# A tile of the fullest expert between the dense stage and the routed one, experts in another order, and another engine waiting for the last stores

## The chip, the cores and the metric

The kernel runs on 1 core of one Trainium2 chip. Its metric is device time in microseconds (us) of one execution. Engines are called PE or TensorE (matmuls), VectorE or DVE, ScalarE or ACT, GpSimd or POOL, and SyncE or SP (which here issues DMAs only).

## The reference

Linear attention without a softmax (4 batches, 8 heads, 576 rows, 64 columns) gives x of 2304 rows by 512. A dense mixture of 4 experts follows, then a routed one of 8 experts with one expert a row:

```python
    for e in range(E):                       # dense: E = 4, F = 1024
        h = np.maximum(x @ w1[e], 0.0)
        out += p[:, e:e + 1] * (h @ w2[e])
...
    logits = xn @ en.T / tau                 # routed: E = 8, F = 1024
    expert_idx = np.argmax(logits, axis=1)
...
    for e in range(E):
        mask = expert_idx == e
        h = np.maximum(x[mask] @ w1[e], 0.0)
        out[mask] = gate_w[mask, None] * (h @ w2[e])
```

By this formula on its inputs (seed 0) the 8 experts get 120, 639, 189, 727, 149, 36, 293 and 151 rows; of the first 1536 rows the fourth expert gets 484.

## The kernel before, in words

Every product keeps nearly full precision by splitting both sides into a high part (fp32r) and the remainder: high times high, high times low and low times high, three matmuls (`three`, L1285).

**Dense stage.** 48 steps (`STEPS`): 3 thirds of 768 rows by 16 units (4 experts by 4 quarters of F). A step's `up` has seven products (a Strassen-like scheme, combined on VectorE in `combine`), then `down` makes six tiles of 128 rows, which VectorE adds to the accumulator `acc` (`add`, L976). GpSimd makes the low parts of the weights. Meanwhile the routed weights are split "ahead" (steps in `AHEAD_AT`) and stored as `parts` in HBM: for each expert eight pieces of 1 MB, four of w1 and four of w2 (`PIECE`, `PCS`).

**Routing.** The 18 tiles of rows are routed in 7 blocks (`BLOCKS`); 4 blocks of 3 tiles inside the dense steps (`ROUTE_AT`), and 3 blocks of 2 in the tail, while the last third's down products run in the order `TAIL`. For a tile: PE transposes it (`flip`, L1367), ScalarE takes the squares (`route`) and copies the transposed rows to `xt`, PE makes logits (`logits`, L1382, one tile at a time; or, inside the steps, `logits_by_tile` and `logits_by_token`, L1392 and L1403, three tiles together), GpSimd the norms (`norms`), VectorE the one-hot (`choose`, L1033), ScalarE the exponentials, PE the rank of each row within its expert (`ranks`, L1414 to L1418), VectorE each row's place (`place`), and GpSimd scatters the rows with an indirect DMA (`scatter`, L551) into `rows` in HBM, a region for each expert.

**Tables.** When all 18 tiles are ranked, VectorE works out tables from the counts (L1112 to L1152): which row each tile begins at (`tab_r`, L1133, first `tab_ready`), which place (expert in use) it belongs to (`tab_o`, L1141, second), the expert of each place and the tiles through each place (third). SP loads two numbers (L410) and issues the rows of tiles 0 and 1 (L413). PE runs small matmuls on the identity in between (`WARM`, L1517, L1520, L1524).

**Routed stage.** A loop over pairs of tiles, as many as the tables say (rounded up to a pair). For a tile PE transposes the rows (`flip_rows`, L1465), multiplies by w1 (`routed_up`, 24 matmuls), transposes the hidden rows (`flip_hidden`, L1499) and multiplies by w2 (`routed_down`, 24). ScalarE and VectorE split what is transposed (`rx`, `rt_parts`, L825, L835, L1158, L1170), VectorE multiplies by the gate (`results`), and GpSimd stores with an indirect DMA (`store`, L615) and fetches the rows of a later tile (`load_rows`, L601). SP loads the weights into two slots, the place's w1 when the last up product of the place two before it is done, and its w2 after its last down product (`load_matrix`, L400). At the end GpSimd waits for the stores:

```python
            for s in range(2):
                pool.wait_ge(stored[s], 16 * ((tiles + 1) // 2))
```

Every engine ends with a closing DRAIN and a barrier, which the profile puts at line 198.

## Time and profile before

| | us |
|---|---|
| median of 3 runs | 1143.15 |
| lowest, highest | 1142.08, 1145.65 |
| profiled execution, its own time | 1145.34 |
| its span, first to last instruction | 1143.8 |
| PE busy | 1119.3 (98%) |
| DVE, POOL, ACT busy | 728.7, 655.3, 456.9 |
| HBM read, written | 170.99 MB, 79.98 MB |

Times in the rows count from the start of the span. "L1112" is line 1112 of the kernel. An idle time in brackets stands with what ended it. Starts of merged rows are those of the first instruction, and matmul ends are modelled, so neighbouring matmuls overlap.

### The profile page before, as it was taken

To read this page: it belongs to the slowest core of one execution; us is meant where nothing else is said; L and a number is where in the kernel's file an instruction comes from. 1 tells how busy PE (TensorE), PEld (TensorE's weight loads), DVE (VectorE), ACT (ScalarE), POOL (GpSimd) and SP (SyncE) were. 2 spreads that over 40 slices of the span, in tenths; PEclk is the share of its full clock that TensorE was granted. 3 is DMA by queue.
4 is the path that set the end of the run, shared out by engine and by line. 5 is a ranking of instruction groups with operands and counts; after the bars stand their busy time and mean duration, and the time that the engine had idled before them with its cause. 6 is when DMAs were issued, how large, how long until landed. Compare 5 with 4: busy or idle time off the path is not lost.

```text
span 1143.8 us, 18712 instructions
## 1 busy us (share of the span) xinstructions
PE 1119.3 (98%) x6210; PEld 985.1 (86%) x6211; DVE 728.7 (64%) x1160; ACT 456.9 (40%) x812; POOL 655.3 (57%) x609
## 2 busy tenths in 40 slices
PE   8999999999999999999999999999989999999996
PEld 8888899998899888999898888999887888888885
DVE  4867888888866788888866788888662222222221
ACT  4783444444434534444434534444222222222220
POOL 2597776899868777799868777777330111111101
PEclk9999999999999999999999999999989999999998
DMA  9945777877612448877612438877469759337960
GB/s 256 271 140 182 267 265 273 285 274 259 228 37 90 139 137 300 293 276 261 217 44 86 155 115 312 284 276 257 155 238 391 265 189 381 140 111 296 360 252 13
DMA packets 102433, 250.87 MB, mean 219 GB/s; under 512 B 8254, under 2 KB 48190, under 8 KB 94171
## 3 DMA queue, kind: packets, MB, share of 16 engines
q1 hardware_dynamic: 97360, 235.18, 59.5%
q0 software_dynamic: 4800, 14.72, 3.5%
q8 instruction: 41, 0.67, 0.2%
q14 instruction: 29, 0.24, 0.1%
q10 hardware_dynamic: 203, 0.05, 0.0%
HBM read 170.99 MB, written 79.98 MB: 219 GB/s over the span
## 4 chain that ended last, share of the span: by engine, by line
PE 90%; DVE 6%; ACT 1%; issue 1%; POOL 0%; DMA 0%; SPq 0%; DVEq 0%; POOLq 0%; ACTq 0%
PE ps L1289 28%; PE ps L1291 27%; PE ps L1290 27%; PE ps L1499 2%; PE ps L1247 1%; DVE x_rows L976 1%; PE ps L1465 1%; DVE hT_lo L958 1%; PE ps L1217 1%; PE ps L1367 1%; DVE attn_rows L897 1%; PE ps L1230 1%; DVE hT_lo L965 1%; PE ps L1258 1%; DVE ahead_lo L984 0%
## 5 line engine op out<-in xcount | busy, mean ns | idle before, releaser
L1289 PE MATMUL ps<-w_hi,hT_hi 128*128 128x512 f32 x576 | 227.0, 394 | 2.1 <-DVE x_rows L976 2.0
L1289 PE MATMUL ps<-x_ops_hi,w_hi 128*128 128x384 f32 x672 | 226.8, 338 | 1.9 <-DVE sum L946 1.9
L1291 PE MATMUL ps<-x_ops_hi,w_lo 128*128 128x384 f32 x672 | 225.8, 336 | 0.0
L1291 PE MATMUL ps<-w_hi,hT_lo 128*128 128x512 f32 x576 | 225.2, 391 | 0.0
L1290 PE MATMUL ps<-w_lo,hT_hi 128*128 128x512 f32 x576 | 225.0, 391 | 0.0
L1290 PE MATMUL ps<-x_ops_lo,w_hi 128*128 128x384 f32 x672 | 224.9, 335 | 0.0
L976 DVE SCALAR_TENSOR_TENSOR x_rows<-ps,dense_probs,x_rows 128x512 f32<-128x512 f32 x270 | 190.2, 739 | 16.9 <-PE ps L1291 16.8
L615 POOL DMA_INDIRECT out_dram<-y_rows,row_ids x22 | 22.6, 1028 | 236.0 <-DVE y_rows L1180 141.5
L495 POOL TENSOR_TENSOR w_lo<-w_raw,w_hi 128x512 fp32r<-128x512 f32 x96 | 146.3, 1543 | 12.3 <-ACT w_hi L709 8.0
L1170 DVE TENSOR_TENSOR rhT_lo<-ps,rhT_hi 128x512 fp32r<-128x512 f32 x44 | 28.4, 687 | 172.0 <-ACT rhT_hi L835 172.0
L1289 PEld LDWEIGHTS ps<-x_ops_hi,w_hi 128*128 128x128 f32 x672 | 126.2, 188 | 6.4 <-DVE sum L946 3.2
L1289 PEld LDWEIGHTS ps<-w_hi,hT_hi 128*128 128x128 f32 x576 | 108.2, 188 | 24.0 <-DVE x_rows L976 3.2
L481 POOL TENSOR_TENSOR w_lo<-w_raw,w_hi 128x512 fp32r<-128x512 f32 x48 | 62.4, 1300 | 114.3 <-ACT w_hi L697 114.1
L1291 PEld LDWEIGHTS ps<-w_hi,hT_lo 128*128 128x128 f32 x576 | 108.1, 188 | 22.9
L1290 PEld LDWEIGHTS ps<-x_ops_lo,w_hi 128*128 128x128 f32 x672 | 126.2, 188 | 1.6
L1291 PEld LDWEIGHTS ps<-x_ops_hi,w_lo 128*128 128x128 f32 x672 | 126.1, 188 | 0.0
L1290 PEld LDWEIGHTS ps<-w_lo,hT_hi 128*128 128x128 f32 x576 | 108.2, 188 | 20.6
L735 ACT ACTIVATE product<-ps 128x384 f32<-128x384 f32 x48 | 23.6, 492 | 247.8 <-PE ps L1291 242.8
L486 POOL TENSOR_TENSOR w_lo<-w_sums,w_hi 128x512 fp32r<-128x512 f32 x96 | 122.0, 1292 | 0.2 <-ACT w_hi L685 0.2
L984 DVE TENSOR_TENSOR ahead_lo<-ahead_raw,ahead_hi 128x1024 fp32r<-128x1024 f32 x64 | 84.5, 1321 | 1.2 <-ACT ahead_hi L760 1.2
L1289 PE MATMUL ps<-w_slots,rxT_hi 128*128 x176 | 71.3, 405 | 0.5 <-issue 0.5
L1289 PE MATMUL ps<-w_slots,rhT_hi 128*128 x176 | 71.3, 405 | 0.0
(204 smaller groups left out, 1996.8 us busy)
## 6 DMA issues: line engine op xcount, KB each, us to landing
w_slots<-split_parts SPq DMA_DIRECT2D x64, 1024.0 KB, 5.8
w_raw<-in_moe_w_dram SPq DMA_DIRECT2D x96, 512.0 KB, 3.6
ahead_raw<-in_moe_w_dram SPq DMA_DIRECT2D x64, 512.0 KB, 7.0
split_parts<-ahead_hi SPq DMA_DIRECT2D x64, 512.0 KB
split_parts<-ahead_lo SPq DMA_DIRECT2D x64, 512.0 KB
row_tile<-dispatched_rows POOLq DMA_DIRECT2D x20, 257.0 KB, 5.7
kv<-in_k_dram SPq DMA_DIRECT2D x16, 288.0 KB, 6.8
kv<-in_v_dram SPq DMA_DIRECT2D x16, 288.0 KB, 7.7
```

The costliest lines, as they stand in the source:

```text
L481: g.tensor_tensor(w1l[s][:, 0:2], w1_raw4[:, :, :, 0:P], w1h[s][:, 0:2].bitcast(F32), ALU.subtract)
L486: last = g.tensor_tensor(w1l[s][:, 3 + m:5 + m].rearrange("p m c n -> p (m c n)"), tsum[:, m:m + 2].rearrange("p m c n -> p (m c n)"), w1h ...
L495: last = g.tensor_tensor(w2l[s][:, c, :], w2raw[:, c, :], w2h[s][:, c, :].bitcast(F32), ALU.subtract)
L615: g.indirect_dma_start(out=out, out_offset=bass.IndirectOffsetOnAxis(ap=ids[:, s:s + 1], axis=0), in_=ys[:, s, :], in_offset=None, bounds_ ...
L735: A(p1[:, :], ps[:, 0, 0:HT], ACT.Copy).then_inc(p1_copied, 1)
L976: V.scalar_tensor_tensor(acc[:, t, 0:D], ps[:, 4 + n % 4, :], pr[:, t, e:e + 1], acc[:, t, 0:D], ALU.mult, ALU.add).then_inc(y_used, 1)
L984: V.tensor_tensor(slo[:, s, :], sraw[:, s, :], shi[:, s, :].bitcast(F32), ALU.subtract).then_inc(s_lo, 1)
L1170: V.tensor_tensor(rhl[:, s, half * 512:(half + 1) * 512], ps[:, 3 + half, :], rhh[:, s, half * 512:(half + 1) * 512].bitcast(F32), ALU.sub ...
L1289: mm(out_, ah, bh, start=(first and m == 0), stop=False, skip_group_check=not final or not first)
L1290: mm(out_, ah, bl, start=False, stop=False, skip_group_check=not final or not first)
L1291: last = mm(out_, al, bh, start=False, stop=(final and m == n - 1), skip_group_check=not final or not first)
L1499: last = tr(ps[:, 3 + half, c * P:(c + 1) * P], hs[:, m:m + P], ident[:, :])
```

## The change

1. **Early tile.** After four blocks (12 tiles) VectorE sorts the experts by count during step 46 (`order_places`). The fullest one (the star) gives its first 128 rows: SP loads them with the star's w1, the first half of its w2 and the first half of the next expert's w1 after the last up product, and the rest of the star's w2 after the last down product. PE's `early_up` and `early_down` process them between the routing's own matmuls and the loop; the fillers are gone. The star's region then counts from 128 rows further on, and the loop's tiles start at number 1.
2. **Alternating places.** The experts are taken in the order fullest, emptiest, second fullest, second emptiest and so on, not by number. The tables get two steps that bring the counts into that order, and three for the expert of a place.
3. **Grouped logits.** Blocks 4 and 5 (the first two in the tail) use `logits_by_tile` and `logits_by_token` for their two tiles; VectorE reads and chooses block 4 after the tail's product 8, before after product 7, and reads block 5 after the last.
4. **The last stores** are waited for by VectorE behind its loop; GpSimd ends behind its own loop.

```diff
+    STAR_AT = 46
+    T0 = TT - TPT
...
+            def load_piece(n, e, m, c):
                 sp.dma_start(W[:, n * PIECE:(n + 1) * PIECE].bitcast(F32),
...
+            def load_early(n, c):
+                sp.dma_start(W[:, n * PIECE:(n + 1) * PIECE].bitcast(F32),
+                             parts[e_star, :, (PCS + c) * PIECE:(PCS + c + 1) * PIECE]).then_inc(early_in[c // 2], 16)
...
-            sp.wait_ge(up_done, OPS * STEPS)
+            sp.wait_ge(star_ready, 2)
+            e_star = sp.value_load(tab_s[0:1, 0:1], min_val=0, max_val=E2 - 1)
+            e_next = sp.value_load(tab_s[0:1, 1:2], min_val=0, max_val=E2 - 1)
+            r_star = sp.value_load(tab_s[0:1, 2:3], min_val=P, max_val=E2 * CAP)
             for s in range(2):
                 sp.wait_ge(s_out[s], 32 * (NAHEAD // 2))
-            for n in range(2 * PCS):
-                load_first(n)
+            sp.wait_ge(scattered, 16 * T0)
+            sp.dma_start(xs[:, 0, :], rows[bass.ds(r_star, P), :]).then_inc(first_rows_in[0], 16)
+            sp.wait_ge(up_done, OPS * STEPS)
+            for c in range(2):
+                load_piece(c, e_star, 0, c)
+            for c in range(2):
+                load_early(PCS + 2 + c, c)
+            for c in range(2):
+                sp.wait_ge(part_in[0][c], 16)
+                load_piece(2 + c, e_star, 0, 2 + c)
+            for c in range(2):
+                sp.wait_ge(part_in[0][c], 32)
+                load_piece(PCS + c, e_next, 0, c)
...
+            for c in range(2, PCS):
+                load_early(2 * PCS + c, c)
...
-            sp.wait_ge(scattered, 16 * TT)
-            for s in range(2):
-                sp.dma_start(xs[:, s, :], rows[bass.ds(first_rows[s], P), :]).then_inc(first_rows_in[s], 16)
-            for s in range(2):
-                sp.wait_ge(first_rows_in[s], 16)
-            for n in range(2 * PCS, 4 * PCS):
-                load_first(n)
+            sp.wait_ge(scattered, 16 * T0)
+            sp.wait_ge(scattered_late, 16 * TPT)
+            sp.dma_start(xs[:, 1, :], rows[bass.ds(first_rows[0], P), :]).then_inc(first_rows_in[1], 16)
+            sp.dma_start(xs[:, 0, :], rows[bass.ds(first_rows[1], P), :]).then_inc(first_rows_in[2], 16)
+            for c in range(2):
+                for half in range(2):
+                    n = (2 * PCS + c) * PIECE + half * PIECE // 2
+                    m = (PCS + c) * PIECE + half * PIECE // 2
+                    sp.dma_start(W[:, n:n + PIECE // 2].bitcast(F32), parts[e_star, :, m:m + PIECE // 2]).then_inc(part_in[1][c], 16)
+            sp.wait_ge(ry_done, 2)
+            for c in range(2, PCS):
+                sp.wait_ge(part_in[0][c % 2], 48)
+                load_piece(PCS + c, e_next, 0, c)
+            for c in range(PCS):
+                sp.wait_ge(part_in[1][c % 2], 32 + c // 2 * 16)
+                load_piece(3 * PCS + c, e_next, 1, c)
...
-            pool.wait_ge(scattered, 16 * TT)
...
-            for s in range(2):
-                pool.wait_ge(rx_done, s + 1)
-                pool.wait_ge(gi_copied, s + 1)
-                load_rows(s + 2, s)
+            pool.wait_ge(rx_done, 2)
+            pool.wait_ge(gi_copied, 2)
+            load_rows(3, 1)
...
-            with pool.Fori(0, PAIRS) as i:
+            for s in range(2):
+                store(s, s)
+                pool.wait_ge(rx_done, s + 3)
+                pool.wait_ge(gi_copied, s + 3)
+                load_rows(s + 4, s)
+            with pool.Fori(1, PAIRS) as i:
...
                             load_rows(2 * i + s + 4, s)
-            for s in range(2):
-                pool.wait_ge(stored[s], 16 * ((tiles + 1) // 2))
...
+            for s in range(2):
+                act.wait_ge(s_out[s], 32 * (NAHEAD // 2))
+            rx(0, 0)
+            for t in range(T0, TT):
                 route(t)
                 if t == TT - 4:
                     exponentials(NB - 3)
+                if t in (T0 + 1, T0 + 3):
+                    copy_by_tile(block_of(t))
...
+            for half in range(2):
+                relu_half(0, half)
+                rt_half(0, 0, half)
...
+            def order_places(part):
+                if part == 0:
+                    dve.wait_ge(rank_read, NB - 3)
+                    step(V.tensor_tensor(ec(0), run[:, :], ebase[:, :], ALU.subtract))
...
+                    V.tensor_copy(tab_s[:, 0:2], order[:, 0:2]).then_inc(star_ready, 1)
+                    V.tensor_copy(tab_s[:, 2:3], starts[:, 0:1]).then_inc(star_ready, 1)
+                    step(V.scalar_tensor_tensor(ebase[:, :], chosen_at[:, 0, :], float(P), ebase[:, :], ALU.mult, ALU.add), False)
+                    step(V.tensor_scalar(jumps[:, E2 - 1:E2], starts[:, E2 - 1:E2], -1.0, float(E2 * CAP + P), ALU.mult, ALU.add))
+                if part == 4:
...
+                        if k == STAR_AT and j < 5:
+                            order_places(j)
...
-                if n == 7:
+                if n == 2:
+                    rx(0, 0)
+                    V.tensor_copy(early_gi[:, :], xs[:, 0, D:D + 2]).then_inc(gi_copied, 1)
+                if n == 8:
                     read_logits(NB - 3)
                     choose(NB - 3)
                 if n == 9:
                     read_ranks(NB - 3)
                     place(NB - 3)
                     gates(NB - 3)
-                if n == 10:
-                    read_logits(NB - 2)
+            read_logits(NB - 2)
...
             step(V.tensor_tensor(ec(0), run[:, :], ebase[:, :], ALU.subtract))
+            step(V.tensor_tensor(cmpo[:, :, :], chosen_at[:, :, :], ec(0).unsqueeze(1).to_broadcast(oe), ALU.mult))
+            step(V.tensor_reduce(ec(0), cmpo[:, :, :], AX.X, ALU.add))
...
+            step(V.tensor_tensor(cmpd[:, :, :], cmpd[:, :, :], ec(9).unsqueeze(1).to_broadcast(ke), ALU.mult))
+            rt_half(0, 0, 0)
             step(V.tensor_reduce(kc_(0), cmpr[:, :, :], AX.X, ALU.add), False)
             step(V.tensor_reduce(kc_(4), cmpd[:, :, :], AX.X, ALU.add))
-            step(V.scalar_tensor_tensor(kc_(5), kc_(3), float(P), kc_(0), ALU.mult, ALU.add))
+            step(V.tensor_tensor(kc_(5), kstart[:, :], kc_(0), ALU.add))
...
             V.tensor_scalar(tab_o[:, :], kc_(1), kcu(2), None, ALU.min).then_inc(tab_ready, 1)
+            rt_half(0, 0, 1)
...
+            def first_results():
+                dve.wait_ge(gi_copied, 1)
+                V.tensor_copy(ids[:, 0:1], early_gi[:, 1:2])
+                dve.wait_ge(ry_done, 2)
+                V.tensor_scalar(ys[:, 0, :], ps[:, 5, :], early_gi[:, 0:1], None, ALU.mult).then_inc(ry_ready, 1)
...
+            for s in range(2):
+                dve.wait_ge(stored[s], 16 * ((tiles + 1) // 2)).then_inc(dve_turns, 1)
...
                 pe.wait_ge(xt_copied, BLOCKS[b][1])
                 pe.wait_ge(c21_done, k + 1)
+                if b:
+                    pe.wait_ge(rank_read, b)
+                first, end = BLOCKS[b]
                 for c in range(KC):
-                    for g in range(3):
-                        last = mm(ps[g * EW:(g + 1) * EW, 3, 0:P], enT[:, c, :], xt[:, g, c * P:(c + 1) * P],
+                    for g in range(end - first):
+                        last = mm(ps[g * EW:(g + 1) * EW, 3, 0:P], enT[:, c, :], xt[:, (first + g) % 3, c * P:(c + 1) * P],
                                   start=(c == 0), stop=(c == KC - 1))
                 last.then_inc(lgt_done, 1)
...
+            def early_up(half, chunks):
+                pe.wait_ge(rx_split, 1)
+                pe.wait_ge(y_used, TPT * STEPS)
+                if half:
+                    pe.wait_ge(lg_read, NB)
+                for c in chunks:
+                    for d in range(2):
+                        pe.wait_ge(part_in[0][d], 16 * (c // (KC // 2) + 1))
+                    cs = slice(c * P, (c + 1) * P)
+                    m = c // (KC // 2) * 2 * PIECE + c % (KC // 2) * F + half * 512
+                    last = three(ps[:, 1 + half, :], [(rxh[:, 0, cs], rxl[:, 0, cs], W[:, m:m + 512], W[:, PIECE + m:PIECE + m + 512])], c == 0, c == KC - 1)
+                if chunks[-1] == KC - 1:
+                    last.then_inc(rh_done, 1)
...
+            def early_down(chunks):
+                half = chunks[0] // (FCH // 2)
...
+                pe.wait_ge(rt_split, half + 1)
+                pe.wait_ge(early_in[half], 32)
...
+                if chunks[-1] == FCH - 1:
+                    last.then_inc(ry_done, 1)
...
             for n, (kk, j) in enumerate(TAIL):
                 down(kk, j)
+                if n == 1:
+                    pe.wait_ge(h_lo, 4 * LAST + 1)
+                    flip_rows(0, 0)
+                if n in (7, 11):
+                    logits_by_token(NB - 3 + n // 11, LAST)
                 if n in (3, 5, 7, 9, 11):
                     flip(T0 + n // 2 - 1, LAST)
-                if n in (4, 6, 8, 10):
-                    logits(T0 + n // 2 - 2, LAST)
+                if n in (6, 10):
+                    logits_by_tile(NB - 3 + n // 10, LAST)
                 if n == 9:
                     ranks(NB - 3, LAST)
             flip(TT - 1, LAST)
             logits(TT - 2, LAST)
             ranks(NB - 2, LAST)
             logits(TT - 1, LAST)
+            early_up(0, (0, 1))
             ranks(NB - 1, LAST)
...
+            early_up(0, (2, 3))
+            early_up(1, (0, 1))
+            pe.wait_ge(rank_read, NB)
+            flip_half(0, 0)
+            early_up(1, (2, 3))
+            early_down((0, 1))
+            flip_half(0, 1)
+            early_down((2, 3))
+            early_down((4, 5))
...
-            for _ in range(2 * WARM):
-                mm(ps[:, 6, 0:P], ident[:, :], ident[:, :], start=True, stop=True)
             pe.wait_ge(tab_ready, 2)
-            for _ in range(WARM // 3):
-                mm(ps[:, 6, 0:P], ident[:, :], ident[:, :], start=True, stop=True)
             tiles = pe.value_load(tab_n[0:1, 0:1], min_val=TT, max_val=KT)
-            flip_rows(0, 0)
-            for _ in range(WARM // 2):
-                mm(ps[:, 6, 0:P], ident[:, :], ident[:, :], start=True, stop=True)
             flip_rows(1, 1)
-            routed_up(0, 0)
-            flip_hidden(0)
-            with pe.Fori(0, PAIRS) as i:
+            early_down((6, 7))
+            flip_rows(2, 0)
+            routed_up(1, 1)
+            flip_hidden(1)
+            flip_rows(3, 1)
+            routed_up(2, 0)
+            e = place_of(1)
+            off = pe.snap((e % 2) * (2 * WCOL))
+            for c in range(2):
+                pe.wait_ge(part_in[1][c], 32)
+            routed_down(1, 1, 0, e, off)
+            flip_hidden(2)
+            routed_down(1, 1, 1, e, off)
+            with pe.Fori(1, PAIRS) as i:
```

**PE's order at the handover, before.** Behind the last logits and ranks stand the fillers (`ps<-ident`), then the rows of tile 0 (`row_tile`):

```order
L1382 MATMUL ps<-enT,xt_route 128x8 [waits c12_done,xt_copied]
L1382 MATMUL ps<-enT,xt_route 128x8 x3
L1414 MATMUL ps<-r_oh,tri 128x16 [waits rank_read,c21_done,oh_ready]
L1416 MATMUL ps<-r_oh,ones 128x8
L1418 MATMUL ps<-r_oh,ones 128x8 x2
L1517 MATMUL ps<-ident 128x128 x24
L1520 MATMUL ps<-ident 128x128 [waits tab_ready]
L1520 MATMUL ps<-ident 128x128 x3
L1521 TENSOR_LOAD table_totals
L1521 ISA x2
L1465 MATMUL ps<-ident,row_tile 128x128 [waits first_rows_in0]
```

**PE's order there with the change.** `xt_route` is the logits' operand, `r_oh` that of the ranks, `w_slots,rxT` the early tile's w1 products:

```order
L1495 MATMUL ps<-enT,xt_route 128x8 [waits c12_done,xt_copied]
L1495 MATMUL ps<-enT,xt_route 128x8 x3
L1403 MATMUL ps<-w_slots,rxT_hi 128x512 [waits routed_w1_in0,routed_w1_in1,y_used,rx_split]
L1404 MATMUL ps<-w_slots,rxT_hi 128x512
L1405 MATMUL ps<-w_slots,rxT_lo 128x512
L1403 MATMUL ps<-w_slots,rxT_hi 128x512 [waits routed_w1_in1,routed_w1_in0]
L1404 MATMUL ps<-w_slots,rxT_hi 128x512
L1405 MATMUL ps<-w_slots,rxT_lo 128x512
L1532 MATMUL ps<-r_oh,tri 128x16 [waits rank_read,c21_done,oh_ready]
L1534 MATMUL ps<-r_oh,ones 128x8
L1536 MATMUL ps<-r_oh,ones 128x8 x2
L1403 MATMUL ps<-w_slots,rxT_hi 128x512 [waits routed_w1_in0,routed_w1_in1,y_used,rx_split]
```

Six of the early tile's matmuls now stand between the last logits and the last ranks, and eighteen more, the hidden rows' transposes and its w2 products take the place of the fillers.

**VectorE's order in the tables, before**, from the comparisons to the row numbers (`table_row_of_tile`):

```order
L1127 TENSOR_TENSOR r_cmpr<-r_cmpk,expert_cols 128x240 [waits r_step]
L1128 TENSOR_TENSOR r_cmpd<-r_cmpd,expert_cols 128x240
L1129 SCALAR_TENSOR_TENSOR expert_cols<-unit,expert_cols 128x8
L1130 TENSOR_REDUCE k_cols<-r_cmpr 128x30 [waits r_step]
L1131 TENSOR_REDUCE k_cols<-r_cmpd 128x30
L1132 SCALAR_TENSOR_TENSOR k_cols<-k_cols 128x30 [waits r_step]
L1133 TENSOR_TENSOR table_row_of_tile<-k_cols 128x30 [waits r_step]
```

**VectorE's order there with the change:**

```order
L1228 TENSOR_TENSOR r_cmpr<-r_cmpk,expert_cols 128x240 [waits r_step]
L1229 TENSOR_TENSOR r_cmpd<-r_cmpd,expert_cols 128x240
L1155 TENSOR_TENSOR rhT_lo<-ps,rhT_hi 128x512 [waits rt_hi,r_step]
L1231 TENSOR_REDUCE k_cols<-r_cmpr 128x30
L1232 TENSOR_REDUCE k_cols<-r_cmpd 128x30
L1233 TENSOR_TENSOR k_cols<-tile_ends,k_cols 128x30 [waits r_step]
L1234 TENSOR_TENSOR table_row_of_tile<-k_cols 128x30 [waits r_step]
```

The subtraction for the early tile's hidden rows (`rhT_lo`), which waits for ScalarE's copy (`rt_hi`), stands in the tables ahead of the row numbers; the scan has moved behind them.

## Rows read from the trace of the kernel before

**Rows 1.** The page: the chain by engine; the stores (count, busy us, mean ns).
```profile
PE 90%; DVE 6%; ACT 1%; issue 1%; POOL 0%; DMA 0%; SPq 0%; DVEq 0%; POOLq 0%; ACTq 0%
...
L615 POOL DMA_INDIRECT out_dram<-y_rows,row_ids x22 | 22.6, 1028 | 236.0 <-DVE y_rows L1180 141.5
```

**Rows 2.** The chain in order of time: start us, us, what.
```profile
615.62 1.00 PE ps L1392 x24
...
829.71 0.79 PE ps L1382 x8
...
852.75 2.68 DMA row_tile<-dispatched_rows
...
875.01 0.87 PE ps L1499 x8
878.69 0.44 PE ps L1465 x4
...
1112.89 0.87 PE ps L1499 x8
```

**Rows 3.** Busy us of each engine by stretch, with the granted clock (PEclk).
```profile
840.50:843.90 3.40, 2.76 (x27) 2.43 (x25) 2.48 (x14) 2.19 (x8) 2.12 (x4) 1.00 0.51 205
843.90:850.70 6.80, 5.20 (x28) 5.21 (x29) 5.70 (x30) 0.61 (x4) 4.04 (x5) 0.50 0.33 126
850.70:857.90 7.20, 6.28 (x54) 5.86 (x53) 3.78 (x19) 0.60 (x1) 0.00 (x0) 1.00 0.47 124
920.00:1000.00 80.00, 80.00 (x382) 65.33 (x381) 17.81 (x36) 18.55 (x32) 9.58 (x12) 1.00 0.66 252
```

**Rows 4.** PE's timeline: start us, us, what, idle time before it and its releaser.
```profile
840.22 0.60 PE L1367 MATMUL ps<-ident,x_rows 128*128 128x128 f32 x4
...
845.50 0.20 PE L1414 MATMUL ps<-r_oh,tri 128*128 128x16 bf16 x1 [1.83 <-DVE r_oh L1033]
...
845.63 8.04 PE L1517 MATMUL ps<-ident 128*128 128x128 f32 x48
...
855.48 0.66 PE L1465 MATMUL ps<-ident,row_tile 128*128 128x128 f32 x4 [0.92 <-DMA row_tile<-dispatched_rows]
855.97 1.50 PE L1524 MATMUL ps<-ident 128*128 128x128 f32 x12
...
857.92 0.50 PE L1289 MATMUL ps<-w_slots,rxT_hi 128*128 x1
```

**Rows 5.** VectorE's timeline, step 47 and the handover.
```profile
813.18 0.56 DVE L946 TENSOR_TENSOR sum<-ps,product 128x384 f32<-128x384 f32 x1 [1.45 <-PE ps L1291]
...
846.91 0.15 DVE L1112 TENSOR_TENSOR expert_cols<-next_row,region_base 128x8 f32<-128x8 f32 x1
...
849.44 0.40 DVE L1128 TENSOR_TENSOR r_cmpd<-r_cmpd,expert_cols 128x240 f32<-128x240 f32 x1
...
850.93 0.19 DVE L1133 TENSOR_TENSOR table_row_of_tile<-k_cols 128x30 int32<-128x30 f32 x1
...
856.80 0.69 DVE L1158 TENSOR_TENSOR rxT_lo<-ps,rxT_hi 128x512 fp32r<-128x512 f32 x1 [2.81 <-ACT rxT_hi L825]
```

**Rows 6.** GpSimd's timeline.
```profile
849.06 0.96 POOL L551 DMA_INDIRECT dispatched_rows<-x_rows,slots  x1 [0.30 <-issue]
859.22 0.59 POOL L601 DMA_DIRECT2D row_tile<-dispatched_rows  x1 [9.20 <-issue]
...
1135.91 0.98 POOL L615 DMA_INDIRECT out_dram<-y_rows,row_ids  x1 [4.62 <-DVE y_rows L1180]
```

**Rows 7.** SyncE's issues, merged: start us, us, what.
```profile
818.31 18.79 SPq L355 DMA_DIRECT2D w_slots<-split_parts  x8
```

**Rows 8.** Line 198, the end of the program: duration ns, start us.
```profile
L198 PEldq DRAIN  x1: 2368/2368/2368, 1131.9 to 1131.9; - x1
...
L198 POOLq DRAIN  x1: 4975/4975/4975, 1138.6 to 1138.6; - x1
```

**Rows 9.** Line 629, GpSimd's wait for the stores.
```profile
L629 POOLq EVENT_SEMAPHORE  x1: 17/17/17, 1138.3 to 1138.3; - x1
```

207 lines of the change are left out of this document (128 added, 79 removed).

## The prediction

> **What bounds the kernel now.** I read the page's chain of waits first: TensorE carries 90% of it, VectorE 6% [rows 1]. I then read that chain in order of time. The reader should see in it that the routed stage is a clockwork: the transposes of the hidden rows come round at 875.01 and, 19 tiles later, at 1112.89 us, so one tile of 128 rows costs (1112.89 - 875.01) / 19 = 12.52 us [rows 2], and in 80 us of that stage PE is busy for 80.00 at the full clock [rows 3]. Nothing is to be won inside the stage except by doing fewer tiles there; 22 are done now, one store each [rows 1].
>
> The third view is PE's timeline where the dense stage hands over. The last down product ends as the transposes of 840.22 begin, and the first routed product starts at 857.92. In these 17.7 us PE waits 1.83 us for the last one-hot, runs fillers on the identity for 8.04 us and more, then waits 0.92 us for the rows from the DMA [rows 4]. The table by stretches shows the clock: 2.4 GHz (1.00) up to 843.90, 1.2 GHz (0.50) for 6.80 us, then full again [rows 3]. What decides this gap is not PE but the chain behind the last block: VectorE starts the tables at 846.91 and has the row numbers at 850.93 [rows 5]; SP loads two of them into registers and issues the rows at 852.75, which land 2.68 us later [rows 2]; GpSimd's last scatter is issued at 849.06 [rows 6].
>
> The last view is the end of the program: the last store is issued at 1135.91 [rows 6], GpSimd's wait for it passes at 1138.3 [rows 9], and then its closing DRAIN takes 4975 ns, from 1138.6 to 1143.6 [rows 8].
>
> **The change, part by part.** *The early tile.* The fullest expert of the first 12 blocks of rows gives its first 128 rows, which are processed between the last down product and the tables. Its region base is moved by 128 rows, so the loop has one tile less: 22 executed in all, 21 behind the handover. That is -12.52 us [rows 2], provided the rest starts no later than 857.92.
>
> Does the gap hold a tile? Its 48 wide products and 8 transposes are 12.52 - 0.44 = 12.08 us [rows 2]; its own row transposes go into the tail. Free in the gap are 1.83 us, the 9.85 us from 845.63 to 855.48, and the fillers from 855.97 up to the second row transposes (857.92 - 0.60 - 855.97 = 1.35): 13.0 us [rows 4]. New in it is a second set of row transposes, 0.44 us. So PE's own work fits with 0.5 us to spare: the first looped product (X below) can't start before about 857.4.
>
> *The path of the rows.* Adding to the tables' chain: two steps that sort the counts by place (0.5 us, between the 0.2 us steps of 8 columns and the 0.4 us ones of 240 [rows 5]), one 128x512 subtraction for the early tile's hidden rows (0.7 us, from a 128x512 step of the same form [rows 5]); leaving it ahead of the row numbers: the used-place flags, their scan and the k+1 column, some 0.5 us. The numbers thus come at 850.93 + 0.7 = 851.6. SP does the same two loads, and its rows land 0.7 us later too, about 856.1 instead of 852.75 + 2.68 = 855.43 [rows 2]. The scatters ahead of them go by the same GpSimd chain as before. Behind the landing PE has the transposes (0.5), six products of the early tile (12.52 - 0.87 - 0.44 = 11.21 for 48, 0.234 each [rows 2], so 1.4), and the next transposes (0.44): X = 858.4. This path, not PE's load, sets X with the clock at full.
>
> *The clock.* In 840.50 to 843.90 PE was busy 2.76 of 3.40 us with short transposes and logits, and the clock then halved until 850.70 [rows 3]. The change leaves these short pieces as they are, and starts the early tile behind them. So I expect part of its first products at 1.2 GHz. Six of them fill the old wait of 1.83 us (1.4 us at full clock, 2.8 at half, so some of it shows); from then on PE is busy without fillers. Bounds: 0, if the clock stays up; and 6.80 / 2 = 3.4 us of lost work, if it is at half for as long as before. VectorE's inserted subtraction waits for this tile, so what PE loses here delays the row numbers. I take +0.8, nearer to the low end, since the stretch from 843.90 had PE busy for little of its first half and for all of its second [rows 3, 4], and now is dense from the start. X = 859.2. The Trainium skill (TensorE: Matmul & The Clock Gate, What's actually happening) says "the default state is throttled, and activity releases the throttle"; the row agrees, the clock fell after transposes and logits and rose after fillers. Taken strictly, it would have the early tile cold from its first product; that is the third rival's case.
>
> *Grouped logits.* Two blocks of two tiles: 8 matmuls of 8 columns a tile at 0.79 us, so 4 x 0.79 = 3.16, become 2 x 16/24 x 1.00 = 1.33 plus two small transposes (0.15 each by my reckoning): 1.5 us saved [rows 2]. The early tile's row transposes take 0.44 back. The choice of block 4 now runs one tile later on VectorE and ScalarE's exponentials stand before the next copy that PE's logits wait for; I estimate 0.5 us for each of two waits. Net 0, bounds -1.1 and +1. The path of the rows starts from the last block, whose order doesn't change.
>
> *Sorting the places* puts 18 small VectorE steps (about 0.2 us, 3.8 us) into step 46. Their cover is the wait of 1.45 us ahead of 813.18 and the smaller ones before it [rows 5], and that no split of routed weights runs there. The sum it must meet has a product of slack besides. I cost it at 0; without the cover it is 0.5 us.
>
> *Weights.* Eight 1 MB pieces took 18.79 us from 818.31 [rows 7], 2.35 each. Eight are still loaded from there, in another order, and two more behind the last down product, which land by about 846 and are used from 853 on. The star expert's first w2 pieces are loaded twice (2 MB, 4.7 us of queue). POOL's row loads share the DMA engines with them; the one at 859.22 [rows 6] has its counterpart in the same distance to X. Cost 0, bound +1.5.
>
> *Alternating places.* By the reference's formula on its inputs the experts have 1, 5, 2, 6, 2, 1, 3, 2 tiles (22). The places become 6 (one early), 1, 5, 1, 3, 2, 2, 2. A place's 8 pieces need 18.8 us, and its slots are free once the place two before it is done, so a place of one tile still leaves two tiles' time. Cost 0.
>
> *The end.* GpSimd no longer waits from the end of its last issue (1135.91 + 0.98 = 1136.9) to 1138.3 and can drain at once: -1.4 us, if the DRAIN is a fixed 4975 ns [rows 6, 8, 9]. PE's DRAIN of 2368 ns began at 1131.9 and ended with its last product, so a DRAIN can also be a wait; but at 1138.6 nothing that the trace shows was under way, which is why I take -1.4; the other end is 0. The Trainium skill (VectorE: DVE Perf Modes, The DRAIN you can't avoid) has the closing DRAINs at about 12 ns on all five engines; the row says 4975 for GpSimd. By the page's figure this part would bring nothing, and by the row 1.4.
>
> **The sum**, on the profiled execution: -12.5 (tile) + 1.3 (X, 859.2 against 857.92) - 1.4 (end) = -12.6 us. Its own time is 1145.34, 2.2 above the median of 1143.15; from the median: **1130.5 us**.
>
> **The rivals.**
> 1. *The DRAIN waits for the store, or ends at a fixed distance behind it.* For it: PE's is such a wait [rows 8]. Then the end gives nothing: 1130.5 + 1.4 = 1131.9. 0.20.
> 2. *The gap is better than my schedule*: clock up, waits overlap, grouped logits pay: X = 857.4 less 0.6 for the tail, 1128.1. Against it: the fall of the clock in rows 3. 0.08.
> 3. *The early tile starts cold and holds the tables up*: 2.5 us more on X, 1133.0, and with a late row load 1134.5. For it: rows 3; 0.14.
> 4. *Weights come late at the places of one tile*: each leaves 18.8 - 12.5 = 6.3 us if loads start one place later than I read; two such places give 1143.1, no change. Against it: today's order has such places too, and no wait shows [rows 2]. 0.03.
> 5. *The other side: the tile is not saved.* If the loop still ran over 22 tiles behind the early one, the total of 23 would be rounded up to the pair, 24: two tiles more, 1130.5 + 25.0 = 1155.5, slower. It decides at the moved region base: the star expert must have 128 rows in the first 12 blocks. It has 484 by the reference, so 0.01.
>
> My forecast itself has 0.54. Of its neighbours rivals 1 to 3 lie close. The range: from 1127.0 (rival 2 and all low bounds) to 1135.5 (rival 3, no gain at the end); it leaves out rivals 4 and 5 and the far tails. A measurement of this kernel tells about 0.3% (3.4 us) from no change; all but the last two cases are faster by more: 0.96, of which I keep 0.01 back for what I haven't seen. Faster 0.95, same 0.035, slower 0.015.
>
> **What would show it.** Right: no fillers, PE busy from the last logits on; the first looped product at 858 to 860; 12.52 us from tile to tile and the last product some 20 such distances behind the first; GpSimd's DRAIN starting near 1126 and still 5 us long; row numbers some 0.7 us later against the last logits. Wrong: waits on weights in the loop; a distance other than 12.52; a VectorE wait for the early tile's hidden rows in the middle of the tables of more than 1 us (then rival 3); a DRAIN that grew by what the wait gave up (rival 1).

## The result, and the profile after

The changed kernel took 1131.73 us (median of 4 runs, 1130.72 to 1132.88) against 1144.4 for the kernel before in the same session (4 runs, 1142.08 to 1145.65): a ratio of 0.9892, 95% interval 0.987 to 0.9914. The forecast was 1130.5 with a range of 1127.0 to 1135.5, and "faster"; it is 1.1% faster. Ten runs of the changed kernel over two sessions have a median of 1133.1 (1130.7 to 1136.0), 48 runs of the kernel before over all sessions 1144.4; that makes 11.3 us, and this is the better number, for a reason that comes below.

The page has PE at 92% of the chain (90 before) and VectorE at 3% (6 before); 22 stores as before, as in [rows 1]:
```profile
PE 92%; DVE 3%; ACT 2%; DMA 1%; issue 1%; POOL 0%; SPq 0%; POOLq 0%; DVEq 0%; ACTq 0%
...
L652 POOL DMA_INDIRECT out_dram<-y_rows,row_ids x22 | 22.1, 1002 | 226.2 <-DVE y_rows L1280 122.8
```

The chain in order of time; to be compared with [rows 2]. The transposes of the hidden rows still come every (1100.51 - 887.67) / 17 = 12.52 us. Ahead of them the chain runs, as it did not before, over the early tile's hidden rows (ScalarE's copy, VectorE's subtraction), VectorE's register load (L1290), its split of the first looped rows, GpSimd's register load and a row load of 6.78 us:
```profile
847.78 0.61 ACT rhT_hi L870
848.48 0.70 DVE rhT_lo L1155
...
855.28 0.55 DVEq L1290
856.21 0.69 DVE rxT_lo L1151
857.10 0.50 POOLq L640
...
858.63 6.78 DMA row_tile<-dispatched_rows
...
887.67 0.87 PE ps L1591 x8
...
1100.51 0.87 PE ps L1591 x8
```

The stretches that answer to [rows 3]; the columns are the same:
```profile
838.00:842.00 4.00, 3.94 (x31) 3.28 (x30) 2.61 (x17) 2.18 (x8) 2.37 (x4) 1.00 0.98 293
842.00:845.50 3.50, 3.50 (x12) 2.27 (x11) 2.83 (x17) 0.60 (x4) 2.05 (x3) 0.51 1.00 413
845.50:850.00 4.50, 4.41 (x21) 3.32 (x20) 3.62 (x13) 1.79 (x3) 2.04 (x2) 1.00 0.63 246
```
The clock is at 1.2 GHz (0.51 as the mean of this stretch) for 3.4 us instead of 6.8, and PE has next to no free time around the last logits and behind them: 3.94 of 4.00, 3.50 of 3.50, 4.41 of 4.50 us.

PE's timeline, to be read against [rows 4]: no fillers, the last logits, the first product of the early tile, the last ranks, the first looped row transposes, the first looped product with the wait ahead of it, and the transposes for the third looped tile with theirs:
```profile
840.07 1.06 PE L1495 MATMUL ps<-enT,xt_route 128*128 128x8 f32 x8
840.98 0.51 PE L1403 MATMUL ps<-w_slots,rxT_hi 128*128 128x512 f32 x1
...
843.02 0.20 PE L1532 MATMUL ps<-r_oh,tri 128*128 128x16 bf16 x1
...
854.30 0.66 PE L1568 MATMUL ps<-ident,row_tile 128*128 128x128 f32 x4
...
857.33 0.50 PE L1403 MATMUL ps<-w_slots,rxT_hi 128*128 x1 [0.50 <-DVE rxT_lo L1151]
```
```profile
865.45 0.66 PE L1568 MATMUL ps<-ident,row_tile 128*128 128x128 f32 x4 [0.93 <-DMA row_tile<-dispatched_rows]
```

VectorE's timeline, against [rows 5]: the first sum of step 47; the last one-hot; the start of the tables; the inserted subtraction with a wait of 0.71 us; the row numbers; the split of the first looped rows:
```profile
809.79 0.55 DVE L1004 TENSOR_TENSOR sum<-ps,product 128x384 f32<-128x384 f32 x1
```
```profile
842.79 0.17 DVE L1092 TENSOR_TENSOR r_oh<-iota_e,r_cols 128x16 bf16<-128x16 f32 x1
...
844.55 0.15 DVE L1214 TENSOR_TENSOR expert_cols<-next_row,region_base 128x8 f32<-128x8 f32 x1
...
848.48 0.69 DVE L1155 TENSOR_TENSOR rhT_lo<-ps,rhT_hi 128x512 fp32r<-128x512 f32 x1 [0.71 <-ACT rhT_hi L870]
...
850.05 0.19 DVE L1234 TENSOR_TENSOR table_row_of_tile<-k_cols 128x30 int32<-128x30 f32 x1
...
856.21 0.69 DVE L1151 TENSOR_TENSOR rxT_lo<-ps,rxT_hi 128x512 fp32r<-128x512 f32 x1 [0.97 <-ACT rxT_hi L862]
```

GpSimd's, against [rows 6], and its closing DRAIN of line 207 (duration ns, start us), against [rows 8]:
```profile
846.71 1.14 POOL L590 DMA_INDIRECT dispatched_rows<-x_rows,slots  x1 [0.31 <-issue]
858.63 0.59 POOL L641 DMA_DIRECT2D row_tile<-dispatched_rows  x1 [10.78 <-DVE gate_and_id L1267]
...
1123.54 0.98 POOL L652 DMA_INDIRECT out_dram<-y_rows,row_ids  x1 [4.62 <-DVE y_rows L1280]
```
```profile
L207 POOLq DRAIN  x1: 4910/4910/4910, 1124.5 to 1124.5; - x1
```

**Where the time went.** I count from the start of the tail: SyncE's first issue of routed weights, which waits for the last dense up product, at 818.31 in the trace before and 814.94 in this one (0.06 for its register move included).

| us | before | changed | difference |
|---|---|---|---|
| start of the program to the start of the tail | 818.31 | 814.94 | -3.37 |
| to the first looped product | 39.62 | 42.39 | +2.77 |
| from there to the last product | 275.93 | 264.14 | -11.79 |
| last y rows to the end | 9.47 | 7.74 | -1.73 |

With the 0.43 between last product and y rows this is the whole difference of the two spans, 1143.76 - 1129.65 = 14.1. The first row is not the change: the dense stage runs the same instructions but for the 18 small steps in step 46, and these cost nothing (from VectorE's first sum of step 47 to the start of the tail it is 818.31 - 813.18 = 5.13 us before [rows 5] and 814.94 - 809.79 = 5.15 now). The difference sits in two VectorE instructions. The line that writes the low half of the hidden rows, in the trace before (min/median/max ns) and its two longest besides one of 2.6 us that both traces have:
```profile
L958 DVE SCALAR_TENSOR_TENSOR hT_lo<-sum,hT_hi x48: 548/654/4355, 78.1 to 817.8; 128x384 fp32r<-128x384 f32 x48
```
```profile
402.71 3.30 DVE L958 SCALAR_TENSOR_TENSOR hT_lo<-sum,hT_hi 128x384 fp32r<-128x384 f32 x1
```
```profile
659.42 4.36 DVE L958 SCALAR_TENSOR_TENSOR hT_lo<-sum,hT_hi 128x384 fp32r<-128x384 f32 x1
```
and in the changed kernel:
```profile
L1016 DVE SCALAR_TENSOR_TENSOR hT_lo<-sum,hT_hi x48: 547/652/2604, 77.9 to 814.3; 128x384 fp32r<-128x384 f32 x48
```
Behind the 3.30 us one the dense steps of the kernel before start 1.3 us later than those of the changed kernel, behind the 4.36 us one another 2.0; the first loads give 0.2, and the small rest is spread. So the profiled pair differs by 14.1 us, of which 3.4 lie ahead of the start of the tail and are chance (after_again shows such a shift in the unedited kernel), and 10.7 are the change.

### The profile page after: what moved, and what is told of

The parts are those of the page before. It is cut to its first block, busy times and chain, and to the rows that moved or that the text cites. A ratio compares the mean times of both kernels' runs of the same rounds, so it can differ in the third digit from the quotient of the medians.

```text
span 1129.6 us, 18534 instructions
## 1 busy us (share of the span) xinstructions
PE 1110.4 (98%) x6144; PEld 972.7 (86%) x6145; DVE 728.1 (64%) x1183; ACT 456.2 (40%) x814; POOL 653.3 (58%) x608
## 4 chain that ended last, share of the span: by engine, by line
PE 92%; DVE 3%; ACT 2%; DMA 1%; issue 1%; POOL 0%; SPq 0%; POOLq 0%; DVEq 0%; ACTq 0%
PE ps L1403 29%; PE ps L1405 28%; PE ps L1404 28%; PE ps L1591 2%; PE ps L1361 1%; PE ps L1568 1%; DMA q<-in_q_dram 1%; PE ps L1483 1%; PE ps L1331 1%; DMA row_tile<-dispatched_rows 1%; PE ps L1508 1%; DVE x_rows L1034 0%; DVE attn_rows L955 0%; PE ps L1372 0%; PE ps L1344 0%
## 5 line engine op out<-in xcount | busy, mean ns | idle before, releaser
L1403 PE MATMUL ps<-w_slots,rxT_hi 128*128 (+1 forms) x176 | 72.0, 409 | 0.9 <-DVE rxT_lo L1151 0.5
L1403 PE MATMUL ps<-w_slots,rhT_hi 128*128 (+1 forms) x176 | 71.7, 407 | 0.1
```

Of the source, the lines that this page charges most:

```text
L1403: mm(out_, ah, bh, start=(first and m == 0), stop=False, skip_group_check=not final or not first)
```

## The experiments

Each kernel ran beside the kernel before on the same chip. In the table every time but the first column's is us behind the start of the tail in the profiled execution; "to the last" is from the first looped product to the last product, "end" from the last y rows.

| kernel | start of tail | last ranks | row numbers | row load issued | first looped product | to the last | end | median of runs |
|---|---|---|---|---|---|---|---|---|
| before | 818.31 | 27.2 | 32.6 | 34.4 | 39.62 | 275.93 | 9.47 | 1144.4 (48) |
| changed | 814.94 | 28.1 | 35.1 | 36.6 | 42.39 | 264.14 | 7.74 | 1131.7 (4) |
| the same again | 816.60 | 28.1 | 35.2 | 36.8 | 42.53 | 264.45 | 7.74 | 1134.8 (6) |
| end_only | 816.00 | 27.2 | 32.6 | 34.4 | 39.63 | 276.83 | 7.82 | 1141.9 (9) |
| half_late | 817.47 | 28.6 | 34.2 | 37.0 | 43.19 | 264.16 | 7.74 | 1134.6 (4) |
| logits_each | 816.96 | 28.6 | 34.9 | 36.4 | 42.16 | 264.23 | 7.74 | 1134.8 (4) |
| rows_early | 815.86 | 28.1 | 35.1 | 36.7 | 41.79 | 262.59 | 7.74 | 1131.7 (4) |
| thin_early | 815.71 | 28.1 | 34.4 | 36.0 | 41.70 | 265.8 | 7.74 | 1133.5 (2) |
| descending | 815.23 | 28.1 | 34.4 | 37.1 | 42.34 | 266.46 | 7.74 | 1134.7 (4) |
| both | 817.10 | 27.9 | 34.1 | 36.5 | 41.73 | 262.58 | 7.74 | 1131.0 (4) |
| both_again | 815.30 | 28.1 | 34.8 | 36.4 | 41.58 | 262.56 | 7.74 | 1129.8 (6) |
| all_three | 818.13 | 27.9 | 33.5 | 36.6 | 41.73 | 262.60 | 7.74 | 1133.3 (4) |
| light_loads | 823.98 | 27.9 | 33.6 | 35.2 | 41.84 | 262.59 | 7.74 | 1133.7 (4) |
| no_last_stores | 816.20 | 28.2 | 35.0 | 36.6 | 42.27 | 264.59 | 1.99 | 1127.3 (2) |

**end_only: VectorE's closing wait alone, on the kernel before.**
```
-            for s in range(2):
-                pool.wait_ge(stored[s], 16 * ((tiles + 1) // 2))
+            for s in range(2):
+                dve.wait_ge(stored[s], 16 * ((tiles + 1) // 2)).then_inc(dve_turns, 1)
```


> The kernel before with one part of the change: VectorE instead of GpSimd waits for the last stores at the end. Theory A (GpSimd's closing DRAIN has a fixed length): it starts right behind the last issue, is again 4.9 to 5.0 us long, and the end from the last product's y rows to the end of the program shrinks from 9.4 to about 7.7 us; the time is 1.4 to 1.8 us below the kernel before. Theory B (the DRAIN waits for the store's transfer or ends at a fixed distance behind it): the DRAIN grows by what the wait gave up, to about 6.5 us, and the time stays. The dense stage of two executions can differ by 3 us from chance stalls, so the distance at the end decides, not the total.


The last y rows on VectorE, and the DRAINs of line 198, in that trace:
```profile
1132.89 0.75 DVE L1178 TENSOR_SCALAR y_rows<-ps,gate_and_id 128x512 f32<-128x512 f32 x1 [4.62 <-PE ps L1291]
```
```profile
L198 POOLq DRAIN  x1: 4992/4992/4992, 1135.5 to 1135.5; - x1
L198 DVEq DRAIN  x1: 17/17/17, 1137.1 to 1137.1; - x1
```
GpSimd drains from 1135.5 on for 4992 ns while its store is still on the way (VectorE's wait for it passes at 1137.1). The end shrinks from 9.47 to 7.82 us; the ratio is 0.9976, interval 0.9966 to 0.9987. The loop has 0.9 us more than in the trace before (276.83), a product that was 0.6 late to issue in one tile; it is in no other trace. Theory A holds, and my first rival falls.

**half_late: the early tile's first subtraction behind the row numbers.**
```
-            rt_half(0, 0, 0)
             step(V.tensor_reduce(kc_(0), cmpr[:, :, :], AX.X, ALU.add), False)
...
             V.tensor_tensor(tab_r[:, :], kc_(5), kc_(4), ALU.subtract).then_inc(tab_ready, 1)
+            rt_half(0, 0, 0)
```


> The changed kernel, with VectorE's subtraction for the first half of the early tile's hidden rows put behind the row numbers instead of ahead of them. Now VectorE sits idle 0.71 us for it and spends 0.69 on it inside the chain of the tables. Theory A (the first looped product is set by the path of the rows): the row numbers come 1.2 to 1.4 us earlier against the last ranks, the rows land as much earlier, and the first looped product starts about 1 us earlier. Theory B (it is set by TensorE's own load): TensorE waits 1 us longer for that half ahead of the early tile's down products, and the first looped product is 0.5 to 1 us later. Both measured from the start of the tail (first weight load behind the last dense up product): now 42.3 us.


GpSimd's last two scatters with the time from issue to landing, SyncE's wait ahead of its row load (L441; us in total, times, longest), and PE at the early tile's first w2 product:
```profile
L590 POOL DMA_INDIRECT dispatched_rows<-x_rows,slots x2: 958/1047/1136, 848.4 to 849.6; - x2
...
DMA to landing us min/median/max: 4.6/4.8/4.9
```
```profile
SPq L441 <- DMA dispatched_rows<-x_rows,slots: 1.2, 1, 1.2
```
```profile
852.55 0.50 PE L1403 MATMUL ps<-w_slots,rhT_hi 128*128 128x512 f32 x1 [1.03 <-DVE rhT_lo L1155]
```
The numbers come 0.9 us earlier behind the start of the tail (34.2), but the row load is issued 0.3 later than in the changed kernel. The load waits for the landing of the last scatter, issued at 849.64 and landed 4.6 us later at 854.24; it goes out at 854.45. Theory A had left this leg out: there is a second one behind the last block, and it is as long as the tables. Theory B came out as written: PE waits 1.03 us for the late subtraction, takes the first looped rows only at 857.57, behind their landing (854.45 + 2.7 = 857.15), and the first looped product is 0.8 later. The clock makes part of this: it fell 1 us earlier than in the changed kernel and held the last ranks back (28.6 instead of 28.1). How the 0.8 divides between the two is open.

**logits_each: the tail's logits ungrouped.**
```
-                if n in (7, 11):
-                    logits_by_token(NB - 3 + n // 11, LAST)
-                if n in (6, 10):
-                    logits_by_tile(NB - 3 + n // 10, LAST)
+                if n in (4, 6, 8, 10):
+                    logits(T0 + n // 2 - 2, LAST)
```
with ScalarE's copies taken out and VectorE's reads put back to where they were.


> The changed kernel with the logits of the tail as before the change: 8 matmuls of 8 columns for each of the four tiles 12 to 15, no grouping, and VectorE's reads and choices in their old places. If grouping pays (my first reckoning was 1.5 us of TensorE saved against two waits of 0.5), the last down product ends about 0.5 us later than now against the start of the tail; if the waits of the copies behind the exponentials eat it, it ends at the same point or up to 0.5 us earlier. TensorE spends 1.5 us more on logits either way. Time of the whole: within 1 us of the changed kernel.


The last down product starts 22.40 behind the start of the tail instead of 22.16, so grouping gains 0.24 up to there, half of what the first theory had; the last one-hot is there at 27.66 instead of 27.85, so it loses that again. The last ranks come 0.5 later all the same, because the clock fell at 25.97 instead of 27.2 and stretched the early tile's six products ahead of them. In return VectorE does not wait ahead of its subtraction, and the row numbers are at 34.9. The first looped product is at 42.16, not later than 42.39 and 42.53. What grouping saves on PE does not reach it. The median, 1134.8, is that of the changed kernel's second session.

**rows_early: three small moves.**
```
+            gates(1, 1)
             step(V.tensor_tensor(cmpo[:, :, :], ec(6).unsqueeze(1)
...
+            rx(1, 1)
             dve.wait_ge(tab_ready, 3)
...
+            r3 = pool.value_load(tab_r[0:1, 2:3], min_val=0, max_val=E2 * CAP + P)
             pool.wait_ge(rx_done, 2)
```


> The changed kernel with three small moves at the handover: VectorE copies gate and id of the first looped tile ahead of its last five table steps, it splits that tile's transposed rows before it loads the number of tiles into a register, and GpSimd loads the row number of the third looped tile before it waits. Theory A (the wait of 0.93 us for the third tile's rows comes from a late issue, which hangs on the gate copy and a register load): the issue is 1.5 to 2 us earlier, the wait is gone, and the first looped product is 0.3 to 0.6 us earlier; together 1 to 1.5 us. Theory B (the wait comes from the DMA queue behind the weight loads, the rows land when these pieces are through): the issue is earlier, the landing stays at 8 us behind the first looped product, and only the 0.3 to 0.6 us remain.


GpSimd's row load in that trace:
```profile
856.62 0.59 POOL L646 DMA_DIRECT2D row_tile<-dispatched_rows  x1 [7.85 <-DVE able_tiles_through_place L1268]
```
It is issued at 40.8 instead of 43.7 behind the start of the tail, and takes 6.8 us to land as in the changed kernel, so it is the issue that was late. The wait of 0.93 is gone, and so are 0.38 us in front of the next w1 product; the stretch to the last product shrinks from 264.14 to 262.59, and the first looped product comes 0.6 earlier: 2.2 us of the profile, more than theory A asked. The medians of four runs (1131.7 and 1131.7) show none of it, since this profile's start of the tail is 0.9 later; see the repeats.

**after_again: the changed kernel, unedited.**


> The changed kernel once more, unedited, in more rounds. Theory A (part of the measured difference is chance in the dense stage, whose executions differ by up to 3.4 us through the first loads and through single VectorE subtractions that take 3 to 4 us instead of 0.65): from the end of the dense up products on, its profile repeats the first one (first looped product 42.4 us behind it, last product 264.1 behind that, 7.74 at the end), while the point from which this counts moves by 1 us or more; the median comes out between 1132 and 1134. Theory B (the dense stage is faster by the change itself): the point stays at 815 and the median at 1131.7.


Each part behind the start of the tail repeats within some 0.3 us, while the start itself moves by 1.66: 0.6 at the first dense step, 1.1 behind a single subtraction of 3.27 us at 403.3. The median is 1134.75, ratio 0.9915 (0.9901 to 0.993), 3 us above the first session's. Theory A, and more of it than I had put on it (1132 to 1134).

**descending: the places by size.**
```
-                    step(V.tensor_scalar(ec(1), ec(0), -2.0, float(2 * E2 - 1), ALU.mult, ALU.add))
-                    step(V.scalar_tensor_tensor(ec(1), ec(0), 2.0, ec(1), ALU.mult, ALU.min))
-                    step(V.tensor_tensor(chosen_at[:, :, :], ec(1)
+                    step(V.tensor_tensor(chosen_at[:, :, :], ec(0)
```


> The changed kernel with the places in order of size (6, one of them early, then 5, 3, 2, 2, 2, 1, 1 tiles) instead of alternating (6, 1, 5, 1, 3, 2, 2, 2). Two VectorE steps in step 46 fall away with it, which were hidden. Theory A (a place's eight pieces of weights need 18.8 us of queue, so two places of one tile behind each other outrun the loads): waits on the weights at the last place, its first pieces 0.5 to 6 us late, and the stretch from the first looped product to the last grows by as much from 264.1 us. Theory B (the pieces are used as they come, a place has two tiles' time, order costs nothing): 264.1 again, and possibly less, since the second place now has five tiles and nothing is pressing behind the handover.


The stretch to the last product is 266.46 instead of 264.14 to 264.45. But the only wait for weights behind 870 us is one of 0.3; 1.7 us come from a fall of the clock that lies elsewhere in this execution, at 866.78, in the middle of the first up products (that stretch by engine, PEclk 0.50):
```profile
866.80:870.20 3.40, 3.09 (x7) 2.48 (x8) 0.69 (x1) 0.56 (x1) 0.00 (x0) 0.50 1.01 422
```
Theory B for the loads: alternating is worth 0.3 to 0.6 us at most on these inputs.

**thin_early: a third of the early tile's products.**
```
-                    last = three(ps[:, 1 + half, :], [(rxh[:, 0, cs], rxl[:, 0, cs], W[:, m:m + 512], W[:, PIECE + m:PIECE + m + 512])], c == 0, c == KC - 1)
+                    last = mm(ps[:, 1 + half, :], rxh[:, 0, cs], W[:, m:m + 512], start=(c == 0), stop=(c == KC - 1))
```
and the same in its down products.


> The changed kernel with only the first of every three products of the early tile: 16 instead of 48, its low parts left out, 7.5 us of TensorE at full clock. Theory A (TensorE's own load sets the first looped product): it comes several us earlier than 42.4 behind the start of the tail, down to what the path of the rows allows. Theory B (the path of the rows sets it, as I forecast): that path still runs through the choice of the last block, the tables and the loads, and only loses the wait for the hidden rows, so the first looped product comes at most 1 us earlier. By the numbers of the trace the row path alone gives: row numbers 4.8 instead of 5.5 us behind the start of the tables, that is 34.0 behind the start of the tail, rows landed 4.2 later, 0.5 + 0.6 + 1.3 + 0.5 behind: 41.1.


```profile
843.79 0.20 PE L1532 MATMUL ps<-r_oh,tri 128*128 128x16 bf16 x1 [1.33 <-DVE r_oh L1092]
...
849.33 1.22 PE L1602 MATMUL ps<-w_slots,rhT_hi 128*128 128x512 f32 x2 [1.40 <-DVE rhT_lo L1155]
...
854.43 1.12 PE L1568 MATMUL ps<-ident,row_tile 128*128 128x128 f32 x4 [0.40 <-DMA row_tile<-dispatched_rows]
```
PE waits again (1.33 for the one-hot, 1.40 for the subtraction, 0.40 for the rows) and the clock is at half for 13.65 us of the gap, so that the row transposes take 1.12 instead of 0.66. The first looped product is only 0.7 earlier, 41.70. Theory B, though its 41.1 was 0.6 too early: without 7.5 us of TensorE's work the path of the rows needs 2.1 us more than before the change. (Its 265.8 to the last product contains another fall of the clock at 867.05.)

**both and both_again: the three moves and the logits ungrouped.** The edits are those of rows_early and logits_each together.


> The changed kernel with the three moves at the handover (gate copy, row split and register load earlier) and the tail's logits ungrouped as in the kernel before. With the moves alone the first looped product came at 41.8 and the stretch to the last product took 262.6 instead of 264.1; with the logits alone it came at 42.2. If the two add, 41.5 + 262.6, that is 2.4 us less than the changed kernel from the start of the tail on; if the clock's fall decides where the ungrouped logits end (it fell 25.97 us behind the start of the tail with them, 27.1 without), they add nothing: 41.8 + 262.6.

> The best version (the three moves at the handover, the tail's logits ungrouped) once more in more rounds. If its gain over the changed kernel is real, the first looped product is again 41.7 us and the end 312.5 us behind the start of the tail, against 314.7 and 315.2 in two profiles of the changed kernel, and the median is 2 us below the 1133.1 us of the changed kernel's ten runs: 1130.5 to 1132. If it was chance in the dense stage, the end is behind the start of the tail by 312.5 all the same but the median is not below 1132.5.


The stretch of the gap in the first of the two, and PE at the first looped rows there:
```profile
837.00:860.00 23.00, 21.14 (x118) 16.46 (x117) 17.29 (x77) 7.11 (x20) 8.37 (x10) 1.00 0.79 282
```
```profile
856.38 0.66 PE L1568 MATMUL ps<-ident,row_tile 128*128 128x128 f32 x4 [0.86 <-DMA row_tile<-dispatched_rows]
```
In the first of them the clock never fell in the gap (PEclk 1.00 from 837 to 860), in the second it fell at 841.89 for 3.4 us as usual. The first looped product is at 41.73 and 41.58, as with the three moves alone (41.79). With the clock up PE waits 0.86 us for the rows, which is the plainest sign that the path of the rows and not PE's load sets the first looped product. The row numbers come 0.8 earlier in this first run than in both_again (34.1, 34.8), but SyncE then waits 0.9 us for the last scatter's landing and issues the rows at 36.5 and 36.4. So in this form the clock decides nothing there, and ungrouping adds nothing to the moves. The end is 312.5 and 312.3 behind the start of the tail, against 314.7 and 315.2 for the changed kernel; ten runs have a median of 1130.5, 2.6 below the changed kernel's ten. The median of both_again alone is 1129.8 (ratio 0.9894), a little under the 1130.5 to 1132 that I expected; the kernel before was at 1143.15 in that session, 1.3 below its 1144.4, so the 2.2 to 2.9 us behind the start of the tail are the firmer number. This is the best version I have, by the moves.

**all_three: and the subtraction late as well.** Edits as in both, plus half_late's.


> The kernel with the three moves at the handover and the tail's logits ungrouped, and besides with VectorE's subtraction for the early tile's hidden rows behind the row numbers, which then come about 0.9 us earlier (33.4 behind the start of the tail instead of 34.3). Theory A (the rows wait for the later of two things, the row numbers and the landing of the last scatter, which came at 36.3 there, and was followed by the row load within 0.2 us): the row load is still issued at about 36.4, right behind the scatter's landing, and the first looped product stays at 41.7. Theory B (the row numbers alone set it): it comes 0.9 us earlier. With A the kernel with the subtraction late is no better anywhere, and the version without it stays the best one.


The last scatter, issued at 849.54, lands 4.9 us later. SyncE's row load:
```profile
854.68 0.33 SPq L442 DMA_DIRECT2D row_tile<-dispatched_rows  x1
```
Row numbers at 33.5, last scatter landed at 854.48, row load 0.2 later, first looped product at 41.73. Theory A, exactly.

**light_loads: 2 MB of weights out of the scatter's way.**
```
-            for c in range(2, PCS):
-                load_early(2 * PCS + c, c)
...
             sp.dma_start(xs[:, 0, :], rows[bass.ds(first_rows[1], P), :]).then_inc(first_rows_in[2], 16)
+            for c in range(2, PCS):
+                load_early(2 * PCS + c, c)
```


> As the kernel with all these moves, but the 2 MB of the star expert's second matrix that are now loaded behind the last dense down product are loaded behind the first looped rows instead; the early tile's last four chunks read its first two pieces again in their place, so its hidden rows 512 to 1023 meet the wrong weights. Theory A (the last scatter lands 3.6 to 5.2 us behind its issue because these 2 MB share the DMA engines with it): it lands within 3.5 us or less, the row load follows the row numbers, and the first looped product comes at 41.0 or earlier. Theory B (the scatter's time is its own): it lands 4 to 5 us behind its issue all the same, and the first looped product stays at 41.7. The rows and the weights behind them may come later by the 4.7 us that the moved 2 MB take, so what follows the first looped product is no gauge.


The last scatters, and PE at the first looped row transposes:
```profile
L590 POOL DMA_INDIRECT dispatched_rows<-x_rows,slots x2: 958/1048/1137, 854.2 to 855.5; - x2
...
DMA to landing us min/median/max: 3.3/3.4/3.6
```
```profile
863.40 0.60 PE L1568 MATMUL ps<-ident,row_tile 128*128 128x128 f32 x4
```
The last scatter lands 3.3 us behind its issue (855.47 to 858.79) instead of 3.6 to 5.2, the row load goes out at 35.2, 1.3 earlier, and the rows are there at 861.84. But PE does not wait for them: it is still in the early tile and takes them at 863.40. The first looped product stays at 41.84. Theory A is right on the scatter and wrong on the product: with the rows early, PE's own load is the next limit, at the same place. Of that load 1.7 us come from a fall of the clock at 850.83, and 0.4 from a wait for the late subtraction; what the rows alone would give with the clock up was not seen.

**no_last_stores: the floor under the end.** GpSimd's loop stores only while another pair of tiles follows, and VectorE's closing wait is for an earlier store.
```
             with pool.Fori(1, PAIRS) as i:
-                with pool.If(2 * i < tiles):
+                with pool.If(2 * i + 2 < tiles):
```


> The changed kernel without the stores of the last two tiles, whose rows are then missing from the output. Theory A (GpSimd's closing DRAIN is a fixed cost that starts when its program ends): it starts at least 20 us before the last product, is again 4.9 us long, and the end comes when the other engines are done, within 1.5 us behind the last y rows instead of 7.74. Theory B (it only ends some time behind the last product or transfer of the program): it stretches to there, or the other engines' closing takes the 5 us as well. By A the end costs 6.2 us more than TensorE needs, only because GpSimd issues the last store.


```profile
1123.50 0.75 DVE L1280 TENSOR_SCALAR y_rows<-ps,gate_and_id 128x512 f32<-128x512 f32 x1 [4.79 <-PE ps L1405]
```
```profile
L207 POOLq DRAIN  x1: 4730/4730/4730, 1108.9 to 1108.9; - x1
```
GpSimd drains at 1108.9, for 4730 ns, beside the last products; that is 14.2 us ahead of the last of them, not 20. The end is 1.99 us instead of 7.74, half a microsecond more than theory A asked. The median is 1127.3 (2 runs). So 5.75 us of every run of the changed kernel are the last store's issue and GpSimd's closing behind it.

## Why the prediction was right, and where it was not

The direction, the size and the range were right, the forecast's 1130.5 by luck: my sum of -12.6 stands against -10.7 behind the start of the tail in the profiled pair, -10.3 in the repeat, and 11.3 in the pooled medians. The first session's -12.7 has some 2 us of chance from the dense stage. Behind the start of the tail I was off by +1.5 at the first looped product, +0.7 in the loop and -0.3 at the end.

- *The early tile, -12.52.* Right: 12.52 from tile to tile, no fillers, one tile less. It was "provided the rest starts no later", and the rest did.
- *The path of the rows, taken as +0.5, and +1.3 with the clock.* This is the term that was mis-sized: 42.39 - 39.62 = +2.77, and +2.9 in the repeat, with the clock's part in it. On the scale of the trace before this is 860.7, outside the 858 to 860 that I had named as the sign of being right. By pieces:
  - The last ranks +0.89, where I had no delay. The six products in the old wait of 1.83 are not the reason: they end at 843.02, just as the one-hot is there, and the ranks follow the one-hot by 0.23 us, before (845.27, 845.50) and now (842.79, 843.02). PE's last logits start later, 25.13 instead of 24.32 behind the start of the tail, and 0.48 of these 0.81 us are there at the last down product. The early tile's row transposes (0.4) stand ahead of it; the rest was not traced. The last logits and the last one-hot before:
```profile
842.63 1.04 PE L1382 MATMUL ps<-enT,xt_route 128*128 128x8 f32 x8
```
```profile
845.27 0.17 DVE L1033 TENSOR_TENSOR r_oh<-iota_e,r_cols 128x16 bf16<-128x16 f32 x1
```
  - From the ranks to the row numbers +1.60. I had 0.7 here for the steps, and they take 0.9. The other 0.71 is VectorE's wait for the hidden rows, and that is the clock's (next but one).
  - SyncE -0.29.
  - From the row transposes to the first product +0.59: the table steps and the register load that VectorE does ahead of the split. I had reckoned this piece from PE's work alone, and it came out slightly shorter than before.

  That it is this path and not PE's load is shown by the run both, where PE waits 0.86 us for the rows, and by thin_early: 7.5 us less work, 0.7 us gained. In the changed kernel itself the two arrive together, the rows landed at 851.58 + 2.7 = 854.28 and PE at 854.30.
- *A leg I left out.* "The scatters ahead of them go by the same GpSimd chain as before" is true of their issue, not of their landing. In end_only, with the old loads, the last scatter lands 3.2 us behind its issue:
```profile
DMA to landing us min/median/max: 3.2/3.2/3.2
```
With two more 1 MB pieces on the queues it takes 3.6 to 5.2. In the changed kernel (3.9) that is covered by the tables; half_late, descending, all_three and the run both, where the numbers are earlier, run into it.
- *The clock, +0.8.* Right in kind and size: it fell for half as long as before, and what PE lost delayed the row numbers, by the 0.71 us that VectorE waits for the hidden rows. In descending, where the clock stayed up here, the same subtraction has no wait, and the row numbers come at 34.4 instead of 35.1:
```profile
848.10 0.69 DVE L1153 TENSOR_TENSOR rhT_lo<-ps,rhT_hi 128x512 fp32r<-128x512 f32 x1
```
  But without the fall the last scatter's landing takes over: descending has its first looped product at 42.34, the changed kernel at 42.39. So the clock's price is in the row numbers and not in the first looped product; the pair both and both_again says the same. (In half_late, where it fell 1 us earlier and held the ranks back, it may have one.) (One reading behind this term was loose: PE was busy for 1.80 of the 3.40 us from 843.90 on, not "for little of its first half".) My schedule's "PE's own work fits with 0.5 us to spare" gives 39.1 behind the start of the tail; light_loads has PE's limit at 41.84, and without the 1.7 us of the clock and the 0.4 of the late subtraction it would be 39.7, an estimate from these rows.
- *Grouped logits, 0.* Right: 0.24 gained at the last down product, 0.19 lost at the last one-hot (logits_each).
- *Sorting the places, 0; weights, 0; alternating places, 0.* Right, with one omission: the row load for the third looped tile. I gave it "the same distance to X" and no cost. It is issued 1.3 us behind the first looped product as before, but then takes 6.78 us, and PE waits 0.93 for it; the step from -12.52 to -11.79 is 0.73. rows_early removes it. The same load in the trace before:
```profile
DMA to landing us min/median/max: 4.9/4.9/4.9
```
- *The end, -1.4.* Right in kind, -1.73 in size: before, the DRAIN began some 1.7 us behind the end of the last issue, not 1.4 (the instructions behind the wait come on top), and now it begins at once. The 12 ns of the Trainium skill (VectorE: DVE Perf Modes, The DRAIN you can't avoid) hold here in kind for VectorE, 17 ns, and not for GpSimd, 4910, nor for PE, whose DRAIN of 2368 ns [rows 8] is a wait; by that figure there was nothing to gain at this point, and end_only gains 1.65.

Rival 1 fell by end_only. Rival 2 (a better gap) fell too: in the run both, with the clock up all through, the first looped product is at 860.0 on the scale of the trace before, and this rival needed 857.4. Rival 3 is half true: a wait of 0.71 for the hidden rows, below the 1 us I had set, and +2.77 at the first looped product where it had +3.8. Rivals 4 and 5 fell. The row numbers against the last logits were to come 0.7 us later and come 1.7 later. The upper bound of my range does not follow from its parts (1133.0 or 1134.5, and 1.4 for the end, give 1134.4 or 1135.9 and not 1135.5); nothing hangs on it. What stays open is the cause of the single long VectorE subtractions (below): no run took GpSimd's work beside them away.

## What to carry to other kernels

Before a stage boundary is filled with work, write down every leg that must end there (here row numbers, the last scatter's landing, PE's load) and not only the one that ends last now: the three came out within a microsecond of each other, and half_late and light_loads, which shortened one or two of them, gained nothing at the first looped product. Compare two executions from a common instant just ahead of the edit; the part before it differed here by more than most terms of the sum. An engine that closes with a fixed DRAIN should not be the one that waits, nor, if it can be helped, the one that issues last.

## What the runs showed of the hardware

- GpSimd's closing DRAIN takes 4.73 to 4.99 us whether the last store has landed (before the change) or is on the way, and runs beside other engines' work.
- A scatter of 128 rows lands 3.2 us behind its issue with no weight loads beside it (end_only), 3.3 with 2 MB of them moved away (light_loads), and 3.6 to 5.2 with them; a row load of 257 KB by GpSimd took 4.9 us before and 6.0 to 7.3 when issued behind four half pieces and up to two whole ones.
- The fall of TensorE's clock at the end of the dense stage took 6.83 us in both traces with the old gap. With the early tile it took 3.41 in eight profiles, from 26.0 to 27.4 us behind the start of the tail; in descending it came only at 51.6, in thin_early it took 13.65, and in both and all_three the clock did not fall.
- Single VectorE subtractions of 128 x 384 with both inputs in SBUF take 2.6 to 4.5 us instead of 0.65, and where they fall differs between executions. Beside the one from 659.42 to 663.78 GpSimd runs these, up to 663.36:
```profile
658.32 2.54 POOL L486 TENSOR_TENSOR w_lo<-w_sums,w_hi 128x512 fp32r<-128x512 f32 x2
660.83 2.53 POOL L495 TENSOR_TENSOR w_lo<-w_raw,w_hi 128x512 fp32r<-128x512 f32 x2
```
The Trainium skill (SBUF — State Buffer, SBUF: two separate sides) has GpSimd and a VectorE operation of two SBUF inputs exclude each other on a shared pair of ports, for a whole instruction; the rows agree with VectorE coming free when GpSimd's row ends, but they are no test of it.
- The first dense step starts up to 6.2 us later from one execution to another (light_loads against the changed kernel; the same instructions up to there). In that window PE waits 4.2 us for the loads of q and v instead of 0.8, so the first loads look like the cause; no run tests it.
